# Attention, routed experts and a gated product on one core: q and k loaded one tile further ahead, rank products in the logits' bank, and the end of the attention stage written out

## What is computed

```
scores = q @ k.T / sqrt(64), masked to 0 <= i - j < 64
attn = exp(scores - max); attn /= sum(attn) + 1e-9;  x = attn @ v
do_compute = x @ w_skip > 0;  e = argmax(x @ w_gate);  g = 1 / (sum(exp(logits - max)) + 1e-9)
x[do_compute] += g * (relu(x @ w1[e]) @ w2[e])
h = x @ w_in;  out = (h * clip(h + 3, 0, 6) / 6) @ w_out
```

## Time and profile before

| what | value |
|---|---|
| median of three runs | 698.8 us |
| profiled execution, its time | 702.35 us |
| profiled execution, its span | 700.7 us |
| TensorE busy over the span | 661.3 us (94%) |
| VectorE, ScalarE, GpSimd busy over the span | 253.0, 241.5, 71.5 us |
| mean granted clock of TensorE | 0.988 |

### The profile page before, as it was taken

One profiled execution on the slowest core, in us unless ns is written; L12 is line 12 of the kernel. 1 busy time (PEld: TensorE's weight loads), 2 busy tenths in 40 slices (PEclk: granted clock), 3 DMA queues, 4 the chain that ended last, 5 costly groups with the idle time before them and its releaser, 6 DMA issues.

```text
span 700.7 us, 17144 instructions
## 1 busy us (share of the span) xinstructions
PE 661.3 (94%) x6662; PEld 581.0 (83%) x6662; DVE 253.0 (36%) x810; ACT 241.5 (34%) x571; POOL 71.5 (10%) x121
## 2 busy tenths in 40 slices
PE   4898787799999999899999999999999999999998
PEld 4687675578787888899999989998999899989996
DVE  2567776411111112465442224222422242233222
ACT  3687767102111212364432223222322232223221
POOL 4223443311111111000000000000000000000000
PEclk9999999799999999999999999999999999999999
DMA  6769969969777172454320002000200020001001
GB/s 149 166 156 214 221 166 299 335 207 382 263 269 267 38 272 81 126 158 136 99 90 1 1 0 91 0 0 0 90 0 0 1 90 0 0 0 45 1 1 45
DMA packets 97251, 78.13 MB, mean 111 GB/s; under 512 B 61793, under 2 KB 76901, under 8 KB 97200
## 3 DMA queue, kind: packets, MB, share of 16 engines
q1 hardware_dynamic: 83392, 43.20, 22.9%
q10 hardware_dynamic: 11360, 30.02, 12.0%
q0 software_dynamic: 2448, 4.22, 1.8%
HBM read 63.23 MB, written 17.52 MB: 115 GB/s over the span
## 4 chain that ended last, share of the span: by engine, by line
PE 81%; DMA 9%; DVE 3%; SPq 3%; issue 2%; ACT 1%; POOLq 0%; POOL 0%; DVEq 0%; ACTq 0%
PE bank L770 29%; PE bank L783 19%; PE av L783 9%; PE bank L733 7%; PE av L744 7%; DMA xin<-x_rows 4%; DMA kraw<-in_k 3%; PE av L625 2%; PE bank L573 2%; SPq L368 2%; PE bank L663 1%; PE bank L639 1%; DVE xall L999 1%; PE av L703 1%; PE av L755 1%
## 5 line engine op out<-in xcount | busy, mean ns | idle before, releaser
L932 ACT ACTIVATE rel<-bank,half 128x384 f32<-128x384 f32 x96 | 55.9, 582 | 185.1 <-PE bank L770 185.1
L1133 DVE SCALAR_TENSOR_TENSOR act<-rel,bank 128x384 f32<-128x384 f32 x96 | 53.2, 554 | 169.9 <-ACT rel L932 169.9
L770 PE MATMUL bank<-xT_hi,wi_hi 128*128 128x384 f32 x384 | 83.3, 338 | 0.8 <-ACT xT_hi L925 0.8
L770 PE MATMUL bank<-xT_hi,wi_lo 128*128 128x384 f32 x384 | 82.8, 337 | 0.0
L770 PE MATMUL bank<-xT_lo,wi_hi 128*128 128x384 f32 x384 | 82.0, 334 | 0.0
L1137 DVE TENSOR_TENSOR g_lo<-act,g_hi 128x384 fp32r<-128x384 f32 x96 | 53.6, 558 | 67.2 <-ACT g_hi L943 67.2
L783 PE MATMUL bank<-wo_hi,g_lo 128*128 128x512 f32 x192 | 76.1, 397 | 0.0
L783 PE MATMUL bank<-wo_hi,g_hi 128*128 128x512 f32 x192 | 76.0, 396 | 0.0
L783 PE MATMUL bank<-wo_lo,g_hi 128*128 128x512 f32 x192 | 75.7, 394 | 0.0
L770 PEld LDWEIGHTS bank<-xT_hi,wi_hi 128*128 128x128 f32 x384 | 68.9, 188 | 7.8 <-ACT xT_hi L925 1.0
L943 ACT CAST g_hi<-act 128x384 fp32r<-128x384 f32 x96 | 49.3, 513 | 65.4 <-DVE act L1133 65.4
(11 more groups left out here) (126 smaller groups left out, 800.4 us busy)
## 6 DMA issues: line engine op xcount, KB each, us to landing
w1s<-in_moe_w ACTq DMA_DIRECT2D x7, 2048.0 KB, 9.2
w2s<-in_moe_w ACTq DMA_DIRECT2D x7, 2048.0 KB, 16.9
qraw<-in_q SPq DMA_DIRECT2D x36, 128.0 KB, 3.3
kraw<-in_k SPq DMA_DIRECT2D x36, 128.0 KB, 3.4
vnow<-in_v SPq DMA_DIRECT2D x36, 128.0 KB, 3.7
x_new<-xall SPq DMA_DIRECT2D x18, 256.0 KB
out<-ot SPq DMA_DIRECT2D x18, 256.0 KB, 2.1
xn<-x_new SPq DMA_DIRECT2D x17, 256.0 KB, 3.4
```

Of the source, the lines that this page charges most:

```text
L770: last = pe.matmul(bank[f % 4][:, 0:GN], a[:, f, c, :], b[:, c, :], start=(n == 0), stop=(n == 3 * DC - 1))
L932: sc.activation(rel[f % 2][:, :], bank[f % 4][:, 0:GN], ACT.Relu, scale=1.0 / 6.0, bias=half[:, :]).then_inc(s_rel, 1)
L1133: dve.scalar_tensor_tensor(out=act[f % 2][:, :], in0=rel[f % 2][:, :], scalar=1.0, in1=bank[f % 4][:, 0:GN], op0=ALU.min, op1=ALU.mult).th ...
```

## The change

Five things change, all in the attention stage.

1. SyncE issues q and k of tile T+3 instead of T+2 in iteration T (and tile 3 before the loop); the two loads of the gate's weights move behind those of v(1) and q, k(4). On TensorE the transposes of tile 2 move from iteration 0 to iteration 1, and those of tile 3 to the end of iteration 1.
2. The loads of expert 1's weights move from ScalarE's stream to the end of SyncE's iteration 17.
3. In TensorE's order the transposes of the probabilities now come before that of the logits, and the rank products come behind the transposes of the output. The ranks of the first four groups lie in bank[5], beside the logits, and not in bank[7].
4. The copied logits (`lgs`) have two buffers.
5. The five iterations after the last tile are replaced by a written-out order on each engine; there the transposes of the output and the logits take banks that the scores or q and k no longer need, and the last group is counted and gated in one interleaved function, `count_and_place`.

The diff, cut to its core:

```diff
@@ sync: order of the loads
-            sp.wait_ge(s_wg0, 1)
-            sp.dma_start(wg[:, :, 0:NE], ...
+            load_qk(3)
             for T in range(1, NT + STORE):
                 if T < NT:
                     load_v(T)
-                if T + 2 < NT:
-                    load_qk(T + 2)
+                if T + 3 < NT:
+                    load_qk(T + 3)
+                if T == 1:
+                    sp.wait_ge(s_wg0, 1)
+                    sp.dma_start(wg[:, :, 0:NE], ...
...
                 if T == NT - 1:
                     for n in range(DC, 2 * DC):
                         weights_piece(sp, 0, n)
+                    load_w1(sp, 1, s_w[1])
+                    load_w2(sp, 1, s_w[1])
@@ tensor: banks and waits
+        def xs_bank(T):
+            return bank[4] if T < NT - 3 else bank[1 if T == NT - 2 else 0]
+        def lp_bank(T):
+            return bank[5] if T < NT - 3 or T == NT - 2 else bank[4]
+        def rk_bank(G):
+            return bank[5] if G < NG - 2 else bank[7]
...
                 pe.wait_ge(s_oh, G + 1)
-                pe.wait_ge(s_x, min(G * GT + 2 * GT, NT))
-                rk = bank[7]
+                if G < NG - 2:
+                    pe.wait_ge(s_prc, 2 * (G * GT + 2 * GT + 1))
+                else:
+                    pe.wait_ge(s_x, NT)
+                    pe.wait_ge(s_rkc, G)
+                rk = rk_bank(G)
...
+                if T >= 2 * GT + 1 and a == 1:          # transpose_pr
+                    pe.wait_ge(s_rkc, (T - 1) // GT - 1)
@@ tensor: order
+            for T in range(NT):
+                scores(T)
                 if T == 0:
                     transpose_qk(1)
+                if T >= 1:
+                    transpose_pr(T - 1, 0)
+                    transpose_pr(T - 1, 1)
+                if T >= 4:
                     transpose_lg(T - 4)
+                if 1 <= T and T + 2 < NT:
+                    transpose_qk(2 if T == 1 else T + 2)
+                if T >= 2:
+                    transpose_xs(T - 2)
                 if T % GT == 1 and T >= 2 * GT + 1:
                     ranks(T // GT - 2)
+                if T >= 3:
                     logits(T - 3)
+                if T >= 1:
                     values(T - 1)
+                if T == 1:
+                    transpose_qk(3)
+            transpose_lg(NT - 4)
+            transpose_pr(NT - 1, 0)
+            transpose_xs(NT - 2)
+            transpose_pr(NT - 1, 1)
+            values(NT - 1)
+            logits(NT - 3)
+            logits(NT - 2)
+            transpose_lg(NT - 3)
+            transpose_lg(NT - 2)
+            transpose_xs(NT - 1)
+            ranks(NG - 2)
+            logits(NT - 1)
+            transpose_lg(NT - 1)
+            ranks(NG - 1)
@@ scalar: the end
+            take_pr(NT - 1, 0)
+            take_pr(NT - 1, 1)
+            take_xs(NT - 3)
+            take_xs(NT - 2)
+            take_logits(NT - 3)
+            take_logits(NT - 2)
+            weigh(NG - 2)
+            take_xs(NT - 1)
+            take_logits(NT - 1)
+            weigh(NG - 1)
@@ vector: count, the last group, the end
             def count(G):
-                if G == NG - 1:
-                    gate(G)
                 dve.wait_ge(s_rk, G + 1)
                 dve.wait_ge(s_oh, G + 1)
+                if G < NG - 2:
+                    dve.wait_ge(s_lgs, G * GT + 2 * GT - 1)
...
+            def count_and_place(G):
+                dve.wait_ge(s_lex, G + 1)
+                dve.tensor_reduce(gsum ...).then_inc(s_gate, 1)
+                dve.wait_ge(s_rk, G + 1)
+                dve.tensor_tensor(rank ...).then_inc(s_place, 1)
+                dve.tensor_scalar_add(gden ...).then_inc(s_gate, 1)
+                dve.tensor_tensor(rsel ...).then_inc(s_place, 1)
+                dve.reciprocal(xall gate ...).then_inc(s_gate, 1)
+                dve.tensor_reduce(psel ...).then_inc(s_place, 1)
+                dve.tensor_tensor(cb ...).then_inc(s_rkc, 1)
+                dve.tensor_tensor(pos ...).then_inc(s_pos, 1)
...
+            take_logits(NT - 4)
+            choose(NG - 2)
+            assign(NG - 2)
+            normalise(NT - 1)
+            take_logits(NT - 3)
+            take_logits(NT - 2)
+            count(NG - 2)
+            place(NG - 2)
+            take_logits(NT - 1)
+            choose(NG - 1)
+            assign(NG - 1)
+            count_and_place(NG - 1)
```

More of the change, by code:

```diff
@@ L139, in attention_moe_mlp_kernel @@
         rsr = sb("rsr", [P, 2, H // 2])
-        lgs = sb("lgs", [P, P])
+        lgs = [sb(f"lgs{i}", [P, P]) for i in range(2)]
         lg = sb("lg", [P, GT, NE + 1])
@@ L209, in attention_moe_mlp_kernel @@
         s_pos = sem("s_pos")
+        s_gate = sem("s_gate")
+        s_place = sem("s_place")
         s_scat = sem("s_scat")
@@ L647, in logits @@
                 pe.wait_ge(s_prc, 2 * min(T + 3, NT))
-                if T == NT - 1:
-                    pe.wait_ge(s_lgs, T)
+                if T >= 2:
+                    pe.wait_ge(s_lgs, T - 1)
                 for c in range(DC):
-                    last = pe.matmul(bank[5][c * LW:(c + 1) * LW, 0:P], wg[:, c, :], xsT[T % 2][:, c, :],
+                    last = pe.matmul(lp_bank(T)[c * LW:(c + 1) * LW, 0:P], wg[:, c, :], xsT[T % 2][:, c, :],
                                      start=True, stop=True)
@@ L657, in transpose_xs @@
                 pe.wait_ge(s_x, T + 1)
-                if T + 2 <= NT:
+                if T < NT - 3:
                     pe.wait_ge(s_prc, 2 * T + 3)
+                elif T < NT - 1:
+                    pe.wait_ge(s_qT, NT)
+                    pe.wait_ge(s_kT, NT)
                 else:
-                    pe.wait_ge(s_xtc, T)
+                    pe.wait_ge(s_xtc, T - 1)
                 for c in range(DC):
-                    last = pe.transpose(bank[4][:, c * P:(c + 1) * P], xall[:, T, c // 2, c % 2 * P:(c % 2 + 1) * P], ident[:, :])
+                    last = pe.transpose(xs_bank(T)[:, c * P:(c + 1) * P], xall[:, T, c // 2, c % 2 * P:(c % 2 + 1) * P], ident[:, :])
                 last.then_inc(s_xt, 1)
@@ L842, in take_logits @@
                 sc.wait_ge(s_lg, T + 1)
-                if T >= 1:
-                    sc.wait_ge(s_lgt, T)
-                sc.copy(lgs[:, :], bank[5][:, 0:P]).then_inc(s_lgs, 1)
+                if T >= 2:
+                    sc.wait_ge(s_lgt, T - 1)
+                sc.copy(lgs[T % 2][:, :], lp_bank(T)[:, 0:P]).then_inc(s_lgs, 1)
             def take_xs(T):
@@ L851, in take_xs @@
                     sc.wait_ge(s_lg, T - 1)
-                sc.copy(xsT[T % 2][:, :, :].rearrange("p c s -> p (c s)"), bank[4][:, :]).then_inc(s_xtc, 1)
+                sc.copy(xsT[T % 2][:, :, :].rearrange("p c s -> p (c s)"), xs_bank(T)[:, :]).then_inc(s_xtc, 1)
             take_q(0)
@@ L856, in _, with weigh @@
                 sc.copy(warm[:, n * P:(n + 1) * P], ident[:, :]).then_inc(s_warm, 1)
-            for T in range(NT + 5):
-                if exists(T - 1, NT):
+            def weigh(G):
+                sc.wait_ge(s_dl, G + 1)
+                sc.activation(lex[:, :, :], ldl[:, :, :], ACT.Exp).then_inc(s_lex, 1)
+            for T in range(NT):
+                if T >= 1:
                     take_pr(T - 1, 0)
                     take_pr(T - 1, 1)
-                if T == NT:
-                    load_w1(sc, 1, s_w[1])
-                    load_w2(sc, 1, s_w[1])
-                if T < NT:
-                    exponents(T, 0)
-                if exists(T - 3, NT):
+                exponents(T, 0)
+                if T >= 3:
                     take_logits(T - 3)
-                if T < NT:
-                    exponents(T, 1)
+                exponents(T, 1)
                 if T == 0:
@@ L1038, in count @@
             def count(G):
-                if G == NG - 1:
-                    gate(G)
                 dve.wait_ge(s_rk, G + 1)
                 dve.wait_ge(s_oh, G + 1)
-                ranks, total = bank[7][:, RK:RK + GT * NE], bank[7][:, RK + GT * NE:RK + (GT + 1) * NE]
+                if G < NG - 2:
+                    dve.wait_ge(s_lgs, G * GT + 2 * GT - 1)
+                ranks, total = rk_bank(G)[:, RK:RK + GT * NE], rk_bank(G)[:, RK + GT * NE:RK + (GT + 1) * NE]
                 then(dve.tensor_tensor(rank[:, :, :], ranks.rearrange("p (t e) -> p t e", e=NE),
@@ L1059, in _ @@
             take_k(0)
-            for T in range(NT + 5):
-                if T < NT:
-                    take_scores(T)
+            for T in range(NT):
+                take_scores(T)
                 if T == 0:
                     take_k(1)
-                if T % GT == 1 and T >= 2 * GT + 1:
-                    count(T // GT - 2)
-                if exists(T - 4, NT):
+                if T >= 4:
                     take_logits(T - 4)
-                if T + 2 < NT:
-                    take_k(T + 2)
+                if 1 <= T and T + 2 < NT:
+                    take_k(2 if T == 1 else T + 2)
@@ L1074, in _ @@
```

(6 more changed lines are left out.)

60 lines of the change are left out of this document (32 added, 28 removed).

## The result

The changed kernel takes 694.15 us (median of 20 runs, 689.28 to 699.04), the kernel before 698.57 (20 runs, 694.76 to 705.90). The ratio is 0.9943, with a 95% interval of 0.9921 to 0.9965: 4.4 us less by the medians, within 1%. The prediction was 683.6 with a range of 676 to 692. The sign was right; the size was a third of the one forecast, and the chance of 0.13 for "within 1%" is the one that came in.

The account below looks back on a forecast made before the run. No engine was full in the attention stage; late k tiles alternated with TensorE's waits for normalising, plus one-hot waits. Start -3.6, loop -8.5 and end -3.1 sum to -15.2 us: 683.6 from the 698.8 median, range 676 to 692.

Parts of the forecast that it names:

- within 1%: Whole kernel: a change under 7 us, about what can be told from none; chance 0.13.
- start and iteration 3, S(4): Up to S(4), the start of iteration 4's score products: start +1.6, k wait gone; 32.4 instead of 36.05, -3.6 us.
- iterations 4 to 16: Attention loop: earlier loads and new TensorE order give 5.37 us an iteration, floor 5.09, clean pace 5.78; -8.5 us.
- end, S(17) to the first expert product: From iteration 17's scores on: written-out order brings the last scatter to +19.7 instead of +23.4; -3.1 us.
- experts: Everything from the first expert product on shifts as a whole with the attention stage; 0 us of its own.
- The 0.6 given back for its landing: Attention's end: the last scatter meets a DMA queue just draining, so 0.6 of the 3.7 us gain is given back.
- 1.7 us to spare: Loop: with loads one tile further ahead, even the latest landing of k fits before its transpose, by 1.7 us.
- 4.0 us after S(T-1): SyncE's queue: six issues at 0.66 us counted from iteration T-1's score start, before 4 to 6.6 us to land.
- one of the signs: SyncE's queue: issues stretched well over 0.66 us would show the prediction wrong.
- The wait of the values for VectorE: Loop: VectorE's count waits for ScalarE's logits copy, delaying normalising and the next values; 0 to 2.6 us.
- The rival of SyncE's queue: Loop: SyncE's queue becomes the bound and holds 5.8 us an iteration; -9.9 us in all, 689; chance 0.20.
- Faster by over 1%: Whole kernel: gain above 7 us, made up of forecast, floor and nearly all of SyncE's rival; chance 0.82.

Follow-up runs that it names:

- after_light: Changed kernel with only an eighth of each weight matrix loaded for experts 3 to 7: 698.6 us, ratio 0.9884 to the kernel before.
- after_again: Changed kernel, unaltered, profiled a second time: 700.29 us.
- ahead_only: Kernel before with only the q and k loads one tile further ahead and the gate loads moved: 693.04 us (0.9908); timed again, 702.35 (0.9945).
- warm: Changed kernel with six idle turns of TensorE instead of four ahead of the first expert tile: 700.37 us, ratio 0.9887 to the kernel before.
- start_warm: Changed kernel with tile 2 transposed in iteration 0 again and six idle turns ahead of the experts: 702.45 us, ratio 0.9922 to the kernel before.
- e1_on_act: Changed kernel with expert 1's weight loads issued from ScalarE's queue again: 702.15 us, ratio 0.9931 to the kernel before.
- start: Changed kernel with q and k of tile 2 transposed in iteration 0 again, loads still further ahead: 702.52 us, ratio 0.9899 to the kernel before.
- before_again: Kernel before, unchanged, profiled a second time: 705.91 us.

## Why the prediction was wrong

The forecast was -15.2 us. The medians give -4.4, the two first profiles -9.0 (702.35 to 693.31). Point by point:

| step | forecast | first pair of profiles | means of all profiles with that code |
|---|---|---|---|
| start and iteration 3, S(4) | -3.6 | -4.5 | -2.1 |
| iterations 4 to 16 | -8.5 | -7.5 | -4.1 |
| end, S(17) to the first expert product | -3.1 | -0.9 | -1.5 |
| experts | 0 | +4.1 | +3.1 |
| last product | 0 | 0 | 0 |
| sum | -15.2 | -8.8 | -4.6 |

The last column: up to S(17), four profiles of the kernel before (the two without experts and with fewer bytes among them, whose code is the same up to there) against five of the changed one; the end without the pair that has no experts, three against four; the experts' first four tiles with all their bytes, two against three (below). The profiles come from several chips, so these means are rough.

**The basis of the sum failed, and it cost 3 to 4 us.** The steps of start and loop took 36.05 and 114.35 of the earlier trace rows as the kernel's own. In four profiles of that code S(4) is 36.05, 33.21, 32.94 and 34.24, and S(17) 114.35, 109.45, 111.47 and 109.80; the one at hand was the longest in both. It lay 3.5 us above the median of the runs shown, and the sum treated that as a shift of everything ("from which the forecast is 683.6"). But 3.0 us of the excess lay in iteration 3 alone, which took 10.05 us there and 6.97 to 7.06 in the other three: its k tile landed after 6.55 us instead of 5.00 to 5.11, and the products behind that wait took 4.55 us at a granted clock of 0.62 instead of 3.0 at 1.00. That wait is the very thing that the change removes, so the excess was counted as gain: the changed kernel has none of it to lose (its iteration 3 takes 5.0 in all five profiles). The last product takes 411.3 us in both first profiles, and the excess can't be there. Taken off the gain instead, the forecast would have been 687.

**What follows doesn't shift as a whole.** This step was put at nothing, and it is +4.1 in the first pair of profiles, +2.6 in the second, and some +2.6 by the times without the experts. The first four expert tiles take 31.6 and 33.0 us in the two profiles of the kernel before and 33.1 and 33.9 with the loads alone; 35.9, 34.6 and 35.8 in the three of the changed kernel, and between 35.0 and 36.7 in all seven others that have its end. With fewer bytes they are 32.0 before and 32.6 after, in one profile each. So it comes with the new end, and two places are seen in it. The first is the first tile at half clock: 9.1 to 9.3 us in seven of the eight profiles with the new end and four idle turns, 7.76 in the eighth (after_light); with the old end 7.75 to 7.88 in four of five and 9.30 in one. All three runs with six turns are free of it. How long TensorE stood behind its four turns doesn't sort the cases: 1.08 us went with half clock (after_again) and 1.84 with full clock (ahead_only). The second is TensorE standing in the fourth tile, from about 28 to 30 us after the first product, in nine of ten profiles with the changed end and all the bytes, for 0.4 to 2.5 us. Taking the first away brought nothing in time that can be told (warm, start_warm), and taking both away wasn't tried; that these two make up the step isn't shown.

**The end: the order was right, its pace was not.** -3.1 was forecast and 0.9 to 1.5 came. From S(17), values(17) were to run from +7.6 to +8.7 and run from +10.55 to +11.70 (112.86 and 114.01 in the chain), 3.0 late. Half of that arises in iteration 17, which was to end at +4.1 and ends at +5.54: its values wait 0.99 us for VectorE's reduction of the logits. Then the logits transpose stands ahead of the transposes of the probabilities and takes its wait of 1.31 for the normalising with it, as forecast; the clock is lower there (0.83 from 104 to 114), and the two transposes and that of x(16) take about 0.85 each, where some 0.43 was reckoned. Positions of group 4 come at +15.1 instead of +12.5, the six scatters at 1.28 each are as forecast, and the last is at +22.5 instead of +19.7. The 0.6 given back for its landing wasn't needed: 3.58 against 3.62.

**The loop: the pace is met where no k is late.** 5.37 an iteration was forecast. In the two profiles with the changed loop and no wait for k (warm and e1_on_act) it is 5.38 and 5.47; in the changed kernel's five profiles, with 0.9 to 4.4 us of such waits, it is 5.44 to 5.80, in the mean 5.62. (5.37 is two fifths of the way from 5.09 to 5.78, not a third; the 0.05 doesn't matter.) The prediction had k arrive with 1.7 us to spare; that failed in one to three tiles of an execution, in all five for tile 15. The step that failed is the issue, not the landing. The issue was put at 4.0 us after S(T-1), which assumes that SyncE stands ready at that moment; the issues that held tile 15 up ended 9.4 to 11.5 us after S(11), because the queue was late with those ahead of them and some were stretched (2.21 us), one of the signs that the prediction named. The late tiles landed in 3.7 to 5.7 us, within the 6.6 reckoned from the earlier trace rows. The wait of the values for VectorE, priced at 0 to 2.6 us, is 1.2 to 4.2 in all profiles with the changed loop. It isn't the one that was priced: the counts wait for ScalarE's copy for 0.9 us in all from S(4) to S(17) of the first profile, but behind the normalising VectorE places the group, makes its gates and masks the next scores before it reduces the logits, from 86.13 to 90.24 in iteration 14 without a stop, and the values wait for that.

**The rival of SyncE's queue** came out about half. Its 5.8 an iteration is met in one profile of five and missed in the others, but the late k tiles are its work, as the chain above shows. SyncE waits for 3.1 us from S(4) to S(17) in the changed kernel and 9.9 in that of before. The Trainium skill, Perfetto Trace Analysis, section What "DMA-bound" means, would now call the loop DMA-bound on the issuing sequencer; the trace agrees that the queue is nearly solid. With the 16 engines at 0.96 and TensorE at 64.5 of 70.8 us, no run here tells which of the three sets the pace of the other iterations.

**The chances.** Faster by over 1% had 0.82. That chance rested on the same basis: by the means of start and loop, -2.1 - 4.1, 7 us could not be reached without the end.

What stays open: why the products of iteration 1 are slower in the changed kernel than with the loads alone, though the same up to there; when the first expert tile gets half the clock; what holds VectorE for 2 us in the reordered end; and whether any version here is faster than the changed kernel, since the intervals of warm (0.9887) and start (0.9899) overlap its own on both chips.

## What to carry to other kernels

When the profiled execution is slower than the median, ask in which waits it is slower before using it as a shift; if they are the waits that the change removes, the excess comes off the gain. A removed wait can come back elsewhere: here the new order without the earlier loads turned waits for VectorE into waits for k. A load reckoned from the event that frees its buffer needs a queue that is free at that moment; here the queue was 4.5 us behind (72.49 against 68.03 for the v load ahead of tile 15). And a stage that ends otherwise can upset what follows: here idle turns counted for the old end.

## What the hardware showed that was not expected

TensorE stood, as it seems for its own instructions, in the midst of a run of equal products: 2.49 us at 161.27 in the changed kernel, with no semaphore to wait for. A packet of the instruction queue comes through the full DMA engines at that time (queue, kind: packets, MB, share of 16 engines, from 161 to 162 us):

```profile
q10 hardware_dynamic: 137, 0.39, 101.2%
q8 instruction: 1, 0.02, 7.0%
```

All nine profiles with the gap have such a packet, in a half microsecond that begins 2.6 to 2.8 us before TensorE goes on, and the later it is, the longer the gap: it begins 2.4 us ahead of a gap of 0.42, 1.9 ahead of one of 0.84, 1.7 ahead of 1.00, 1.4 ahead of 1.26, 1.1 ahead of 1.54, and 0.3 to 0.7 ahead of those of 2.06 to 2.49. In the two profiles of the changed kernel without the gap the packet comes early enough: 3.7 us before TensorE reaches that place with all the bytes (after_again, 161.5 and 165.2) and 3.1 with fewer (after_light, 162.0 and 165.1). Shorter stands in the second expert tile, 0.2 to 1.6 us in nine of these ten profiles and 0.49 in one of the kernel before (before_again), show the same: such a packet 2.5 to 3.0 us before TensorE goes on. That the packet ends the wait is inferred from this; no run moved the code alone. The Trainium skill, Runtime: NRT & Kernel Launch, section Instruction fetch mechanics, says that each sequencer fetches its code by a DMA queue of its own in blocks of 16 KiB and that this is mostly hidden; the packet's 0.02 MB agrees, and if the inference holds, it was not hidden here, behind weights.

The granted clock fell after some such stands and not after others. It fell to 0.62 and 0.53 at the first expert tile after 1.7 us without a product, and to 0.50 in the fourth tile after 2.1 us in warm and start_warm, where that cost about as much again as the wait. It stayed at 1.00 in the fourth tile in the other seven of the nine profiles, after the 2.49 us of the changed kernel too. No run here shows what decides it.
